# Expert tiles gathered one step further ahead, the next input tile split earlier, and a slot table without the large expert's tokens

## The reference

```python
logits = x @ w_gate + modality_bias[modality_id]
e_idx = np.argmax(logits, axis=1)
gate_w = softmax(logits)[np.arange(N), e_idx]
for e in range(E):
    mask = e_idx == e
    h = np.maximum(x[mask] @ w1[e], 0.0)
    out[mask] = gate_w[mask, None] * (h @ w2[e])
```

## Time and profile before

| | |
|---|---|
| median of 3 runs | 640.39 us (639.28 to 641.01) |
| the profiled execution | 639.25 us |
| its span, from the first to the last instruction | 637.5 us |
| PE busy | 602.2 us (94% of the span) |
| DVE / ACT / POOL busy | 301.4 / 232.5 / 161.4 us |
| mean granted clock of TensorE | 0.981 of full |
| chain that ended last | PE 74%, issue 11%, POOL 6%, DMA 3% |

### The profile page before, as it was taken

How to read it: one execution, slowest core, us unless ns; L and a number is a source line. 1 busy time by engine, 2 the same in 40 slices (tenths; PEclk the granted TensorE clock), 3 DMA queues, 4 the chain that set the end, 5 groups by cost and what they waited for, 6 DMA issues and landing times.

```text
span 637.5 us, 11405 instructions
## 1 busy us (share of the span) xinstructions
PE 602.2 (94%) x3637; PEld 489.9 (77%) x3638; DVE 301.4 (47%) x711; ACT 232.5 (36%) x728; POOL 161.4 (25%) x167
## 2 busy tenths in 40 slices
PE   5999999989999999999999999968999998999994
PEld 3677767668887887878888789946998976788893
DVE  5999999766555855565656233501211200021210
ACT  3888888733333333433343322101212211112210
POOL 5555655530100012224222001371011011101001
PEclk9999999999999999999999999977999998999998
DMA  9876666100000440000000000000096035000000
GB/s 183 189 177 158 161 168 171 36 0 18 33 16 17 141 173 18 16 16 33 16 16 25 9 17 31 33 1 19 20 353 234 20 133 199 18 15 31 14 16 33
DMA packets 70684, 47.51 MB, mean 75 GB/s; under 512 B 56424, under 2 KB 58568, under 8 KB 70656
## 3 DMA queue, kind: packets, MB, share of 16 engines
q1 hardware_dynamic: 68080, 41.36, 22.8%
q0 software_dynamic: 2576, 5.79, 2.5%
HBM read 37.53 MB, written 10.39 MB: 75 GB/s over the span
## 4 chain that ended last, share of the span: by engine, by line
PE 74%; issue 11%; POOL 6%; DMA 3%; DVE 2%; SPq 2%; ACT 1%; POOLq 0%; DVEq 0%; ACTq 0%
PE bank L981 16%; PE pair L966 15%; PE pair L568 15%; PE bank L568 15%; POOL work L540 4%; PE pair L1551 4%; PE pair L1074 2%; DMA xT<-x_dram,g_idx 2%; POOL w_lo L547 1%; PE bank L1094 1%; PE pair L1541 1%; SPq L414 1%; DMA arena<-in_k 1%; PE pair L1106 1%; PE pair L689 1%
## 5 line engine op out<-in xcount | busy, mean ns | idle before, releaser
L966 PE MATMUL pair<-x_lo,lead_hi 128*128 128x256 f32 x288 | 81.5, 283 | 1.6 <-issue 1.6
L966 PE MATMUL pair<-x_hi,lead_hi 128*128 128x256 f32 x288 | 82.3, 286 | 0.5 <-issue 0.3
L966 PE MATMUL pair<-x_hi,lead_lo 128*128 128x256 f32 x288 | 81.5, 283 | 0.0
L1456 POOL TENSOR_TENSOR rstd<-ln_small 128x1 f32 (+1 forms) x18 | 25.4, 1412 | 176.6 <-DVE ln_small L635 176.6
L760 ACT ACTIVATE work<-pair,neg_max 96x128 f32<-96x128 f32 (+2 forms) x176 | 61.5, 368 | 18.3 <-PE bank L700 14.7
L1037 POOL DMA_INDIRECT out<-work,lead_sidx x18 | 17.9, 992 | 189.6 <-ACT work L1021 158.1
L568 PE MATMUL pair<-w_hi,x_hi 128*128 128x512 f32 x144 | 59.7, 414 | 1.4 <-DVE x_lo L657 0.4
L540 POOL TENSOR_TENSOR work<-work,row_inv 96x512 f32<-96x512 f32 (+3 forms) x48 | 44.7, 931 | 53.8 <-DVE row_inv L848 53.8
L568 PE MATMUL bank<-w_hi,lnT_hi 128*128 128x512 f32 x144 | 56.4, 391 | 1.1 <-DVE lnT_lo L1268 1.1
L568 PE MATMUL pair<-w_hi,x_lo 128*128 128x512 f32 x144 | 56.6, 393 | 0.0
L966 PEld LDWEIGHTS pair<-x_hi,lead_hi 128*128 128x128 f32 x288 | 55.2, 192 | 1.4 <-issue 0.8
(11 more groups left out here) (201 smaller groups left out, 1225.4 us busy)
## 6 DMA issues: line engine op xcount, KB each, us to landing
entry<-in_moe_w SPq DMA_DIRECT2D x12, 1024.0 KB, 13.5
arena<-in_q SPq DMA_DIRECT2D x32, 144.0 KB, 2.9
arena<-in_k SPq DMA_DIRECT2D x32, 144.0 KB, 3.2
x_dram<-work SPq DMA_DIRECT2D x18, 256.0 KB, 2.0
arena<-in_moe_w SPq DMA_DIRECT2D x8, 512.0 KB, 7.4
arena<-in_v SPq DMA_DIRECT2D x16, 144.0 KB, 2.5
work<-in_v SPq DMA_DIRECT2D x16, 135.0 KB
arena<-in_moe_w_in SPq DMA_DIRECT2D x8, 256.0 KB, 3.2
```

Source lines behind the costliest of these rows:

```text
L966: ins = pe.matmul(lead_h_ps[n % 2][:, jj * BLK:(jj + 1) * BLK], a[:, w], b[:, x], start=(passes == 1), stop=(passes == 3 * KC))
L1456: pool.tensor_tensor(rstd[:, bass.ds(t, 1)], var_eps, minus_half, ALU.pow).then_inc(rstd_ready, 1)
```

## The change

Three edits. (1) `place()` adds 1,000,000 to the table row of every token of the leader, by two more small DVE operations, and the 18 table DMAs get a bounds check that lets such rows go. (2) In the dense stage `split_x(t+1)` moves on ACT to before `exp_h(t)`, and `rest_x(t+1)` on DVE to before the wait for that exponential. (3) In the expert loop DVE makes the index of gather s+2 before `take_y(s)`, and POOL issues gather s+2 before scatter s, with `gather(1)` ahead of the loop; one gather more than before is made in all.

```diff
--- before.py
+++ after.py
@@ -615,14 +615,14 @@
                 dve.wait_ge(solu_link, n)
 
             solu_t = first_or(t, solu0, solu)
+            if inside(t, -1) and not (static(t) and t == 0):
+                rest_x(dve, t + 1)
             dve.wait_ge(eh_ready, t + 1)
             link(dve.tensor_scalar(sume_h, sum_h, EPS_SUM, None, ALU.add), 5 * t + 1)
             link(dve.reciprocal(inv_h, sume_h), 5 * t + 2)
             wait(dve, ln_turned, 2 * t)
             link(dve.scalar_tensor_tensor(out=solu_t, in0=first_or(t, h_ps0, h_ps)[:, :], scalar=inv_h,
                                           in1=first_or(t, e_h0, e_h), op0=ALU.mult, op1=ALU.mult), 5 * t + 3)
-            if inside(t, -1) and not (static(t) and t == 0):
-                rest_x(dve, t + 1)
             if at(t, NT - 1):
                 lead_rest_x(dve, 0, 0)
                 lead_rest_x(dve, 0, 1)
@@ -1229,6 +1229,8 @@
                 if inside(t, 1):
                     round_ln(t - 1, 0)
                     round_ln(t - 1, 1)
+                if inside(t, -1) and not at(t, 0):
+                    split_x(act, t + 1)
                 if inside(t, 0) and not at(t, 0):
                     exp_h(act, t)
                 if at(t, NT - 1):
@@ -1240,8 +1242,6 @@
                 if at(t, NT + 1):
                     lead_round_h(act, 0, 3)
                     take_logits(4)
-                if inside(t, -1) and not at(t, 0):
-                    split_x(act, t + 1)
                 if piece(t) is not None:
                     round_lead(piece(t))
                 if at(t, SNAP + 2):
@@ -1327,6 +1327,8 @@
                 step(dve.tensor_scalar(rank_i[:, NT:2 * NT], rank_i[:, 0:NT], 7, None, ALU.logical_shift_right))
                 step(dve.tensor_copy(rank_hi, rank_i[:, NT:2 * NT]))
                 step(dve.tensor_scalar(row_base, tok_rev[:, :], -float(T), float(E * T), ALU.mult, ALU.add))
+                step(dve.tensor_scalar(lead_far, tok_rev[:, :], id_rev, FAR, ALU.is_equal, ALU.mult))
+                step(dve.tensor_tensor(row_base, row_base, lead_far, ALU.add))
                 step(dve.scalar_tensor_tensor(out=row_base, in0=rank_f, scalar=float(NT), in1=row_base,
                                               op0=ALU.mult, op1=ALU.add))
                 dve.scalar_tensor_tensor(out=tab_idx[:, :], in0=rank_hi, scalar=1.0 - P * NT, in1=row_base,
@@ -1476,7 +1478,8 @@
             for t in range(NT):
                 pause(pool)
                 pool.indirect_dma_start(out=slot_tab, out_offset=bass.IndirectOffsetOnAxis(ap=tab_idx[:, t:t + 1], axis=0),
-                                        in_=tok_pair[:, 2 * t:2 * t + 2], in_offset=None).then_inc(tab_written, 16)
+                                        in_=tok_pair[:, 2 * t:2 * t + 2], in_offset=None, bounds_check=E * T - 1,
+                                        oob_is_err=False).then_inc(tab_written, 16)
 
 
         def n_pairs(eng):
@@ -1643,8 +1646,8 @@
             stage_gather(1)
             stage_scatter(0)
             with dve.Fori(0, tiles_total(dve)) as s:
+                stage_gather(s + 2)
                 take_y(s)
-                stage_gather(s + 2)
                 stage_scatter(s + 1)
 
             with dve.Fori(ENTRIES_AT, BLOCKS - 1) as o:
@@ -1672,8 +1675,9 @@
             gather(0)
             lead_block_pool(pool, ENTRIES_AT - 1)
             total = tiles_total(pool)
+            gather(1)
             with pool.Fori(0, total) as s:
-                gather(s + 1)
+                gather(s + 2)
                 scatter(s)
 
             with pool.Fori(ENTRIES_AT, BLOCKS - 1) as o:
@@ -1682,7 +1686,7 @@
 
             pool.wait_ge(scattered, 16 * total)
             pool.wait_ge(lscattered, 32 * BLOCKS)
-            pool.wait_ge(gathered, 16 * (total + 1))
+            pool.wait_ge(gathered, 16 * (total + 2))
             pause(pool)
 
         block = ctx.enter_context(nc.Block())
```

## The result

The changed kernel takes 633.9 us (median of 4 runs, 632.63 to 634.72) where the kernel before takes 640.16 (4 runs, 639.28 to 641.01): ratio 0.9901, 95% interval 0.9878 to 0.9923. That is 6.3 us less, where 23 were forecast, and it is the number of the first rival (633.9). That it meets this number to the tenth is luck: the rival added 6.5 us for the other parts, which gave 8.5, and the dip took 1.7 back. The profiled execution has 632.63 us and a span of 630.8.

A forecast was written before the change was run, and what follows sets the result against it. PE's own stream was taken to bound the kernel, busy 94% of the span. Dip 16.5, gathers 4.2 and split 2.3 sum to 23.0 us, from the median 640.39 to 617.4, said as 617; range 614 to 634.5.

The forecast's parts named there:

- the first rival: The dip stays because the same 18 DMAs with as many descriptors crowd out other engines: 633.9 us, chance 0.27.
- the other parts: Gathers ahead and split ahead, the two edits besides the table edit: 6.5 us together.
- The dip: Large expert's block 2, 38.9 us, 16.5 too long during POOL's table DMAs; letting the leader's rows go would close it.
- Theory B: From the experiments' expectations: the dip belongs to the place in the program, the first pass of the loop over blocks.
- Gathers: Expert tiles: the second gather issued 9 us earlier removes PE's 2.53 us wait and the slower down product, 4.2 us.
- Split: Dense stage: earlier x_hi and x_lo shorten PE's step at seven boundaries, 2.3 us; at the others PE doesn't wait.
- Table edit: Two extra DVE operations and 0.3 us of bounds checks on POOL stay hidden; 2180 of 2304 little writes go.

The follow-up runs named there:

- the moved run: The changed kernel with POOL's 18 table DMAs issued one block later, behind the scatters of block 2: 621.34 us, on a chip without the dip.
- rows16_b: The changed kernel with all 18 table DMAs, each over 16 tokens instead of 128, on a chip with the dip: 635.27 us.
- spaced_b: The changed kernel with a POOL operation between each two table DMAs, 1.85 us apart on average, on a chip with the dip: 615.56 us.
- the first pair: The first measurement of the changed kernel against the kernel before: 633.9 against 640.16 us, ratio 0.9901.
- the five groups: Five sets of follow-up kernels, each on one chip beside the kernel before, which took 624.95, 623.18, 641.67, 622.96 and 624.45 us.
- split_only: The kernel before with the move of the input split alone (edit 2), on a chip with the dip: 638.26 us, ratio 0.9936.
- gather_only: The kernel before with the gathers one step ahead alone (edit 3), on a chip with the dip: 636.63 us, ratio 0.9927.

## Why the prediction was wrong

**The dip, 16.5 us: the step that failed.** "I take 'all', for the crawl follows the burst of tiny writes in time and nothing else in that burst is rare in this kernel." Two things were rare, the tiny writes and 18 DMAs without a pause, and I credited the writes. The row against it stood in the same part: POOL's work per DMA would not change (0.958 and 0.973 us), and it did not: the spacing of 1.26 us became 1.28, and the block kept its length. The Trainium skill's rule in the prediction ("DMA: Bandwidth & Descriptors", section "Anatomy of one DMA": about 2.0 us fixed, plus bytes over 436e3) gives a table DMA about 2.0 us however few its bytes. In the DMA list above they land 2.1 us after issue, so the trace agrees. The rule is about the transfer's own time; whether this time is what held the other engines up, no run here shows.

The runs put the spacing in the place of the writes. 1.15 us apart with an eighth of the rows, the excess is 20.7 us; 1.28 us apart, 18.1; 1.26 us apart, 16.5, 17.0 and 18.9 in three traces; 1.85 us apart on average, none. Among the dense runs the excess differs by 2.4 us at one and the same spacing, so no trend is to be read between 1.15 and 1.28. The spaced kernel is one execution on a chip with the dip, and all 26 executions of kernels with a dense run on that chip took 633.6 to 643.6 us, as with a dip. Theory B alone doesn't fit this: on one chip, the same place in the program has the dip or not by the spacing. That a dense run slows the engines only in this place, the first round of the loop over blocks, isn't refuted: the moved run met no dip to move.

**What lies behind it stays open.** The rival's "same number of descriptors" is wrong too, by `rows16_b`. What didn't change with the rows is each DMA's 16 completions, and the lost records of such increments, on just the chips with the dip, fit an overload of whatever carries such events. That is argued, not shown, and a loss of records does not make a dip by itself: `spaced_b` loses 122 of 288 and has none. Nor can it be told whether recording the events has a part in it: each of these runs is known by its profile, with its span and clock, and none was made to see the kernel without one.

**That the dip is not in every set of runs** no row of one trace could say. It is there in 2 of 6 sets (the first pair and the five groups), and the kernel before takes 640 to 642 us in these and 623 to 625 in the rest (medians). Within a set every execution of a kernel with a dense run has it, or none. I call that a property of the chip, but no chip is known to have come up twice, so it could also be one of the occasion. Against that the ratio of the change moves little: 0.9901 with the dip on both sides, 0.9858 and 0.9892 without.

**The dip's 1.7 us more** (40.57 instead of 38.91) I can't put to the bounds check. `split_only` has the old table and 41.37 us, `gather_only` 39.42. The long ones are those with the earlier split, but single traces don't show why. Some 0.7 us of it, by my estimate, is clock: behind the last hole PE went on at half the granted clock for 4.5 us before the change (435.04 to 439.50) and for 5.9 us after it (431.07 to 436.94), and half of each is lost.

**Gathers, forecast 4.2 us: right.** 4.43 in the traces, 4.7 for the edit alone. The gather went out 1.5 us after `turn(1)` began (518.15 to 519.66), as I had it (520.54 to about 522), and neither the weight load nor the scatter behind it in POOL's stream got in the way. One reading was off: in the trace of before the granted clock is still 1.00 in the wait and falls to 0.50 only behind it, from 538.5 to 541.9 us, which is why the down product and not the wait shows the price.

**Split, forecast 2.3 us: right in kind, half in size.** 4.06 in the traces, 4.1 alone. The term was mis-sized in two ways. "At the other boundaries PE doesn't wait" was wrong: I had looked for steps over 0.42 us, and five more boundaries have steps of 0.27 to 0.42 us. And at each boundary I counted one step only, while the next is long as well, 0.32 instead of 0.23. Two of these steps in the trace of before, one at a boundary that I had left out and one behind a boundary that I had counted:

```profile
183.16 0.39 PE L568 MATMUL bank<-w_hi,lnT_lo 128*128 128x512 f32 x1
183.57 0.49 PE L568 MATMUL pair<-w_hi,x_hi 128*128 128x512 f32 x1
...
260.23 0.49 PE L568 MATMUL pair<-w_hi,x_hi 128*128 128x512 f32 x1
260.55 0.39 PE L568 MATMUL pair<-w_lo,x_hi 128*128 128x512 f32 x1
```

Over the seven boundaries the second steps add 0.7 us to the 2.3, and the five others give 1.0: 4.0 in all. The better measure was the period of a whole tile: from 254.70 us on, the maximum of the next tile starts 12.63 to 12.67 us after the last in the trace of before (12.51 at the last tile), and 12.25 us after it now.

**Table edit.** Its costs were hidden as said. That it is worth nothing is shown where there is no dip; with the dip no run tries it alone, and in the changed kernel it closed nothing. The sum, put right: 4.1 + 4.4 + 0 = 8.5 us, against 8.6 and 6.9 measured on the two chips without a dip (the second with an interval of 4.7 to 8.8), and 6.3 to 6.6 on the first, where the dip took 1.7 back.

## What to carry to other kernels

Before a hole in a trace becomes a term of a sum, look at the same kernel in another set of runs, on another chip, above all if nothing that the profile shows releases the waiting engine. When two things set a stretch apart, price the edit with each as the cause: here, on a chip with the dip, thinning the DMAs left the dip as it was, and spacing them gave 19.7 us over that (635.27 thinned, 615.56 spaced, one execution each), for 0.6 us of otherwise useless POOL work behind each of 18 DMAs. And for many small waits of the same kind, compare the period of the whole tile, not the one step that stands out.

## What the runs showed that I had not expected

Eighteen indirect DMAs from POOL, 1.15 to 1.28 us apart, slow PE and ACT on some chips so far that a block of 22.4 us takes 39 to 43, while the DMA engines are 2% busy. On those chips PE's mean granted clock falls to 0.64 in the middle of it, a mix of its two levels, 2.4 and 1.2 GHz; on the others the same run passes beside a full PE at clock 1.00.

The clock is not the cause. In the trace of before PE's first hole ends at 418.18 us, and PE has 11 matmul records in the 5.3 us from 417.0 to 422.3 at clock 1.00; only at 422.44 does the clock fall to its lower level, up to 439.50. After the change the holes begin at 413.44 and the clock falls at 416.46.

The crawl has a step. In the five traces with the dip most starts of PE in it lie 0.70 us apart or 1.40, 2.10 or 2.80, at either clock and with table DMAs 1.15 or 1.28 us apart. So PE is let on at a beat that belongs neither to its clock nor to POOL's DMAs. What beats, the runs don't show.

The likely best kernel of this study is the changed one with spaced table DMAs: 614.3 to 616.1 us on the chips without a dip, the same as the changed kernel alone (614.6 to 616.1), and 615.6 on the one with it. There it would beat both, but that last number is a single execution.
